# Ending a kernel's engine block in a barrier of semaphores alone, without GpSimd's drain

## What is computed

```python
scores = np.where(mask, scale * q @ k.T + bias, -1e9)     # window 128
x = softmax(scores) @ v                                    # 2304 x 512
r = np.maximum(x @ w_in, 0.0)                              # 512 x 2048
x = (s * (r * r) + b) @ w_out                              # 2048 x 512
noisy_logits = x @ w_gate + np.log1p(np.exp(x @ w_noise)) * noise
top2 = np.argpartition(-noisy_logits, 2, axis=1)[:, :2]    # and softmax over the two
for e in range(E):
    for k in range(2):
        mask = top2[:, k] == e
        h = np.maximum(x[mask] @ w1[e], 0.0)               # 512 x 1024
        out[mask] += top2_w[mask, k, None] * (h @ w2[e])
```

## Time and profile before

| | us |
|---|---|
| median of 3 runs | 1105.16 |
| lowest and highest | 1104.12, 1105.37 |
| the profiled execution's own time | 1104.22 |
| its span, first to last instruction | 1102.4 |

### The profile page before, as it was taken

How to read it: one execution, slowest core, us unless ns; L and a number is a source line. 1 busy time by engine, 2 the same in 40 slices (tenths; PEclk the granted TensorE clock), 3 DMA queues, 4 the chain that set the end, 5 groups by cost and what they waited for, 6 DMA issues and landing times.

```text
span 1102.4 us, 18178 instructions
## 1 busy us (share of the span) xinstructions
PE 1048.3 (95%) x5846; PEld 920.0 (83%) x5847; DVE 656.6 (60%) x1955; ACT 479.8 (44%) x988; POOL 118.8 (11%) x124
## 2 busy tenths in 40 slices
PE   5699699999999999999999999999999999999995
PEld 4488598889988888988989879888988889888894
DVE  6877566767776676664476745554645535545422
ACT  6766455546555555543445324332423323233211
POOL 0000000020020020002020211112121111211211
PEclk9899989999999999999999999999999999999998
DMA  6569952242242243213356425352522525323312
GB/s 180 151 221 333 343 182 89 87 162 87 87 154 87 77 126 115 78 39 116 97 189 203 152 80 176 97 166 83 177 95 80 198 80 180 124 83 114 119 38 96
DMA packets 79673, 147.04 MB, mean 133 GB/s; under 512 B 12268, under 2 KB 12908, under 8 KB 79600
## 3 DMA queue, kind: packets, MB, share of 16 engines
q1 hardware_dynamic: 70640, 125.91, 36.2%
q0 software_dynamic: 8960, 20.21, 5.3%
HBM read 108.53 MB, written 46.78 MB: 141 GB/s over the span
## 4 chain that ended last, share of the span: by engine, by line
PE 84%; DVE 5%; ACT 3%; issue 2%; DMA 2%; SPq 2%; POOL 0%; DVEq 0%; ACTq 0%; POOLq 0%
PE bank L1307 21%; PE bank L1309 21%; PE bank L1308 21%; PE bank L1448 8%; PE bank L1288 3%; PE bank L1275 2%; DMA stage_a<-in_w_second 2%; PE bank L1333 1%; PE bank L1456 1%; PE bank L1254 1%; DVE x_sc L843 1%; PE bank L1394 1%; SPq L378 1%; PE bank L1255 1%; PE bank L1401 1%
## 5 line engine op out<-in xcount | busy, mean ns | idle before, releaser
L1307 PE MATMUL bank<-w_hi,g_hi 128*128 128x512 f32 x312 | 127.7, 409 | 1.2 <-DVE g_lo L1189 1.2
L1309 PE MATMUL bank<-w_hi,g_lo 128*128 128x512 f32 x312 | 122.4, 392 | 0.0
L1308 PE MATMUL bank<-w_lo,g_hi 128*128 128x512 f32 x312 | 121.8, 390 | 0.0
L675 ACT ACTIVATE relu<-bank 128x384 f32<-128x384 f32 x96 | 47.0, 490 | 163.6 <-PE bank L1309 163.3
L898 DVE SCALAR_TENSOR_TENSOR relu<-relu,sb_scale 128x384 f32<-128x384 f32 x96 | 59.2, 617 | 70.7 <-ACT relu L675 70.6
L535 POOL DMA_INDIRECT rows_scratch<-x,slot x36 | 38.6, 1073 | 537.7 <-DVE x L979 528.6
L765 ACT ACTIVATE g_hi<-bank 128x384 fp32r<-128x384 f32 x56 | 27.5, 492 | 141.4 <-PE bank L1309 141.4
L615 ACT ACTIVATE x_sc<-x_sc,least 128x256 f32<-128x256 f32 (+1 forms) x144 | 69.9, 488 | 18.3 <-DVE least L843 18.0
L892 DVE TENSOR_TENSOR w_now_lo<-stage_a,w_now_hi 128x1024 fp32r<-128x1024 f32 x48 | 58.7, 1223 | 28.4 <-ACT w_now_hi L669 28.2
L1156 DVE SCALAR_TENSOR_TENSOR g_lo<-bank,g_hi 128x384 fp32r<-128x384 f32 x56 | 31.1, 556 | 72.7 <-ACT g_hi L765 72.4
L843 DVE CUSTOM_DVE_ANT_0 x_sc<-bank,nbias 128x256 f32<-128x256 f32 (+1 forms) x144 | 52.8, 404 | 32.3 <-PE bank L1255 24.6
(11 more groups left out here) (212 smaller groups left out, 2770.4 us busy)
## 6 DMA issues: line engine op xcount, KB each, us to landing
stage_a<-in_w_first SPq DMA_DIRECT2D x92, 256.0 KB, 3.0
stage_a<-in_w_second SPq DMA_DIRECT2D x92, 256.0 KB, 3.1
qk_raw<-in_qk SPq DMA_DIRECT2D x144, 128.0 KB, 2.9
y_scratch<-x SPq DMA_DIRECT2D x21, 768.0 KB, 6.1
stage_b<-in_w_first SPq DMA_DIRECT2D x28, 256.0 KB, 2.8
stage_b<-in_w_second SPq DMA_DIRECT2D x28, 256.0 KB, 3.3
rows_scratch<-x SPq DMA_DIRECT2D x24, 258.0 KB, 8.8
rows<-rows_scratch SPq DMA_DIRECT2D x8, 774.0 KB, 6.7
```

The lines of the kernel that those rows point to most:

```text
L675: act.activation(relu[:, (t * C1 + c) % GR, :], h_bank[c % 2][:, 0:TOK1], ACT.Relu).then_inc(relu_ready, 1)
L1307: pe.matmul(psum, lh, rh, start=(first and n == 0), stop=False)
L1308: pe.matmul(psum, lh, rl, start=False, stop=False)
L1309: done = pe.matmul(psum, ll, rh, start=False, stop=(last and n == len(pairs) - 1))
```

## The change

The block is opened with a flag. It changes what the program has where the block closes, and nothing else: the instructions of all five engines ahead of that place are the same and in the same order.

```diff
-        with nc.Block() as block:
+        with nc.Block(no_gpsimd_drain=True) as block:
```

## The result

The changed kernel took 1094.23 us in the median of four runs (1092.60 to 1095.55), the one before 1104.64 in four (1101.93 to 1105.37, the three known ones among them). The ratio is 0.9914, with a 95% interval of 0.9891 to 0.9936. That is faster by 9.5 us, under 1%, with 7.1 to 12.0 us by the interval. The 7.1 us that were forecast are the interval's lower edge.

The account below looks back on a forecast made before the run. The prediction took GpSimd's 10.18 us drain at the block's end as the bound, with SP next: 1095.0 + 0.1 + 0.2 = 1095.3 against 1102.4, 7.1 us off the 1105.16 median, stated as 1098.0; range 1096.9 to 1105.8 for 8 in 10.

Parts of the forecast that it names:

- What bounds the exit: At the block's end, GpSimd's 10.18 us drain arrives last at 1102.2; without it SP, at 1095.0, sets the end.
- The sum of the exit: Span end: SP's arrival 1095.0 + 0.1 for its new instruction + 0.2 barrier = 1095.3 against 1102.4, gain 7.1 us.
- SP's added instruction: Semaphore instruction behind SP's drain at the block's end, on the path: 0.02 us from below, 0.1 from above, 0.1 taken.
- The landing's spread: Last output scatter's landing, 2.8 us here, now sets SP's arrival: could be 0.1 us earlier or 1.4 us later.
- The reading of the drain's time: GpSimd's final drain: 7.5 us after the last landing are spent by the drain itself, on the descriptor queues' state.
- Points (a) to (c): On GpSimd's drain: 0.188 us at kernel start; 7.5 us more after data landed; no scatter work left on its cores.
- rival C: Behind the barrier, a later drain pays only the unhidden part, 7.5 us after landing: 1105.6 or 1105.2, same; chance 0.15.
- B: Behind the barrier, launch-closing code drains GpSimd and pays the whole 10.18 us: 1108.3, 3.1 us slower; chance 0.13.
- The step that failed: From gain to time range: runs' 1104.12 to 1105.37 less 7.1, plus landing spread, gave 1096.9 to 1099.7.

## Why the prediction was right in its mechanism and wrong in its number

*What bounds the exit.* Right. The last arrival was GpSimd's drain, SP was 7.2 us ahead of it, and SP is now last, in the order and with the waits that were named.

*The sum of the exit, 7.1 us.* Right. In the trace it is 12.04 less 4.95 = 7.1 us, and in 6 runs against 22 it is 7.2 by the ratio (4.6 to 9.6 by its interval).

*SP's added instruction, 0.02 to 0.1 us.* It stands at 1093.3 behind the drain at 1093.2, and the release follows in the next tenths, as taken.

*The landing's spread, 0.1 us earlier to 1.4 later.* The landing at this place was 2.8 us again in the kernel with early drains, and the waits of SP kept their lengths. The upper bound wasn't needed.

*The reading of the drain's time.* "The drain itself, on the descriptor queues' state" was right as far as it went. Points (a) to (c) excluded the data and the scatter's own work. "It isn't waiting for data" holds for this drain, not for drains in general, as line 62 showed. What I didn't see is that the price is a count: 0.082 us for each DMA since the last drain. The 7.5 us "left after the landing" in rival C are no part of their own; the 9.2 us run from 1092.97 on, whenever the scatter lands.

*Rivals B and C.* Both wanted the distance between the time and the span to grow, from 1.8 to 12 or 9 us. It is 1095.3 - 1093.5 = 1.8 us, as before. No later drain pays for the work left undone, within the measured time. The start of the changed kernel shows GpSimd's drain short as well, as in the earlier trace rows, though the record doesn't say whether an execution of the same kernel stood ahead of it:

```profile
L1591 POOLq DRAIN  x1: 187/187/187, 0.3 to 0.3; - x1
```

The rule of the Trainium skill (VectorE: DVE Perf Modes, section The DRAIN you can't avoid), drains on all five engines that come from the launch's preamble and postamble, made B or C the outcome. The measurement decides against that reading: if there is a GpSimd drain behind the barrier, it isn't one that works off the 112 DMAs in measured time. Where that work goes isn't shown, and it may lie outside the measured time.

*The step that failed* is the one from the gain to a time with a range: "the runs span 1104.12 to 1105.37". Three runs were taken for the spread of the kernel, and so all that lies ahead of the exit was taken to repeat within 1.3 us. It didn't: 1.8 us of the difference between the two first profiles lie there. The fourth run of the same kernel was 1101.93. On chip A 22 runs lay within 1102.99 to 1108.91, a breadth of 5.9 us, and on chip B 23 runs within 1098.41 to 1103.12, a breadth of 4.7. The spread goes with the granted clock: a stretch like the one at 543.0 above, at the lower level inside the work, costs 1.7 us. On chip B the runs of the kernel before with a mean clock under 0.982 had a median of 1102.2 (6 runs), those at 0.982 and over 1099.8 (17 runs). The 10.4 us between the two first medians are 7.1 from the exit and 3.3 from ahead of it. That these 3.3 are chance, the four first runs of the changed kernel falling on its quick side, is supported by two independent comparisons, 0.9935 and, with the drain hidden, 0.9944, whose intervals overlap with the first one's, 0.9891 to 0.9936. It isn't shown run by run, because one execution of each kernel was profiled. And the fourth run alone wouldn't have saved the range: 1101.93 less 7.1 and 0.1 is 1094.7, still above 1094.23.

## What to carry to other kernels

Look behind the last piece of work in a trace: an engine's drain isn't busy time, and a chain of work can end long before the span does. What a barrier's slowest arrival costs is its distance to the second slowest, not its own length. For a kernel whose GpSimd issues many DMAs, that drain grows with their number; either leave it out where another engine has waited for every landing, or put drains into GpSimd's idle stretches, which gained as much here within the intervals and keep one at the end. For the range of a forecast, a spread read from three runs is too small.

## What was new about the hardware

- GpSimd's drain took 0.05 us + 0.082 us for each DMA it had issued since its last drain: 0.12 to 0.13, 0.37, 1.34 and 5.27 us for 1, 4, 16 and 64, and the same 1.34 us for 16 of 2 KB as for 16 of 1 MB.
- It also waits for landings: 3.03 us with one scatter still to be issued and to land, where 0.13 was its price once landed. With 112 DMAs the landing added nothing, with 43 the drain ended 1.8 us behind it.
- It is stateful: a second one at once took 0.04 us. A launch that ended without it didn't pay for it elsewhere within the measured time: 1.8 us beside the span, before and after.
